# Seven half-block products in place of eight in the last projection of a fused attention, MoE and FFN kernel

## What is computed

```python
def _moe2_ref(x, w_in, w_out):          # x: 2304 x 512
    h = np.maximum(x @ w_in, 0.0)       # 2304 x 2048
    return (h * h @ w_out)              # 2048 x 512 -> 2304 x 512
```

## Time and profile before

| what | value |
|---|---|
| median of 3 runs | 428.07 us (425.8 to 428.68) |
| the profiled execution's own time | 425.84 us |
| its span | 423.9 us |
| PE busy | 405.3 us, 96% of the span |
| DVE busy | 243.0 us, 57% |
| ACT busy | 218.4 us, 52% |
| granted TensorE clock, mean | 0.986 |

### The profile page before, as it was taken

One profiled execution on the slowest core, in us unless ns is written; L12 is line 12 of the kernel. 1 busy time (PEld: TensorE's weight loads), 2 busy tenths in 40 slices (PEclk: granted clock), 3 DMA queues, 4 the chain that ended last, 5 costly groups with the idle time before them and its releaser, 6 DMA issues.

```text
span 423.9 us, 7956 instructions
## 1 busy us (share of the span) xinstructions
PE 405.3 (96%) x2879; PEld 310.7 (73%) x2879; DVE 243.0 (57%) x679; ACT 218.4 (52%) x559; POOL 98.1 (23%) x94
## 2 busy tenths in 40 slices
PE   5899999999989999799899999999999999999996
PEld 5678787878767654233678888888888888888884
DVE  4788888888845451113999545454545445454520
ACT  2989898989853310002966434344444434344420
POOL 4686868686730010000142000000000000000000
PEclk9899999999999999969999999999999999999999
DMA  7588998998616899999300101010101001010101
GB/s 188 156 293 243 265 298 244 301 283 226 221 32 201 284 378 398 408 386 387 141 2 1 51 0 51 0 49 2 50 2 40 9 0 49 0 49 2 49 0 49
DMA packets 51426, 61.34 MB, mean 145 GB/s; under 512 B 27584, under 2 KB 35264, under 8 KB 49856
## 3 DMA queue, kind: packets, MB, share of 16 engines
q1 hardware_dynamic: 50064, 60.37, 42.8%
q10 hardware_dynamic: 1328, 0.52, 0.5%
HBM read 56.16 MB, written 4.72 MB: 144 GB/s over the span
## 4 chain that ended last, share of the span: by engine, by line
PE 85%; DMA 5%; ACT 5%; DVE 4%; issue 1%; SPq 0%; ACTq 0%
PE psum L1314 15%; PE psum L1315 15%; PE psum L1316 15%; PE psum L1028 6%; PE psum L1072 6%; PE psum L1054 5%; DMA ring<-in_moe_w 4%; PE psum L1295 4%; PE psum L1222 3%; ACT probs L829 3%; PE psum L1243 2%; PE psum L987 2%; PE psum L1132 2%; PE psum L1037 2%; PE psum L1009 2%; PE psum L1170 1%
## 5 line engine op out<-in xcount | busy, mean ns | idle before, releaser
L1314 PE MATMUL psum<-wout_hi,act_hi 128*128 128x512 f32 x288 | 113.3, 393 | 1.7 <-DVE wout_lo L752 1.4
L1315 PE MATMUL psum<-wout_lo,act_hi 128*128 128x512 f32 x288 | 112.9, 392 | 0.0
L1316 PE MATMUL psum<-wout_hi,act_lo 128*128 128x512 f32 x288 | 112.1, 389 | 0.0
L778 DVE TENSOR_TENSOR sq_h<-relu_h 128x512 f32<-128x512 f32 x72 | 56.4, 783 | 77.6 <-ACT relu_h L935 77.5
L935 ACT ACTIVATE relu_h<-psum 128x512 f32<-128x512 f32 x72 | 43.1, 599 | 91.6 <-PE psum L1295 85.7
L829 ACT ACTIVATE probs<-probs,row_min 128x256 f32<-128x256 f32 (+1 forms) x128 | 60.1, 470 | 12.4 <-DVE row_min L563 12.3
L504 POOL TENSOR_TENSOR probs<-probs,row_inv 128x1024 f32<-128x1024 f32 x31 | 59.2, 1930 | 23.7 <-DVE row_inv L614 23.7
L1316 PEld LDWEIGHTS psum<-wout_hi,act_lo 128*128 128x128 f32 x288 | 54.1, 188 | 11.9
L1314 PEld LDWEIGHTS psum<-wout_hi,act_hi 128*128 128x128 f32 x288 | 54.1, 188 | 11.7 <-issue 1.9
L1315 PEld LDWEIGHTS psum<-wout_lo,act_hi 128*128 128x128 f32 x288 | 54.3, 189 | 8.8
L782 DVE TENSOR_TENSOR act_lo<-sq_h,act_hi 128x512 fp32r<-128x512 f32 x72 | 49.8, 692 | 5.9 <-ACT act_hi L938 0.6
(11 more groups left out here) (141 smaller groups left out, 439.4 us busy)
## 6 DMA issues: line engine op xcount, KB each, us to landing
ring<-in_moe_w SPq DMA_DIRECT2D x16, 1024.0 KB, 6.1
ring<-in_moe_w SPq DMA_DIRECT2D x4, 2048.0 KB, 13.5
out_x<-out_sb SPq DMA_DIRECT2D x9, 512.0 KB, 2.8
v_in<-in_v SPq DMA_DIRECT2D x32, 128.0 KB, 2.8
ring_late<-in_moe_w SPq DMA_DIRECT2D x2, 2048.0 KB, 8.6
ring_x<-in_moe_w SPq DMA_DIRECT2D x2, 2048.0 KB, 7.9
win_sb<-in_moe_w_in SPq DMA_DIRECT2D x4, 1024.0 KB, 14.2
wout_raw<-in_moe_w_out SPq DMA_DIRECT2D x4, 1024.0 KB, 14.4
```

The costliest lines, as they stand in the source:

```text
L778: nc.vector.tensor_tensor(sq_h[:, u % 2, :], relu_h[:, u % 2, :], relu_h[:, u % 2, :], ALU.mult).then_inc(sq_done, 1)
L1314: mm(to, hi, wout_hi[:, c, :], start=first_of, stop=False)
L1315: mm(to, hi, wout_lo[:, c, :], start=False, stop=False)
L1316: last = mm(to, lo, wout_hi[:, c, :], start=False, stop=last_of)
```

## The change

From group 3 (`CONV`) to group 8, a group's projection (256 tokens x 2048 by 2048 x 512) is cut into halves on all sides: tokens in two halves of 128, hidden columns in two halves k of 1024, output columns in two halves of 256. Of these half blocks seven products are made instead of eight, in the scheme of Strassen and Winograd. Four are of sums: S1 to S4 are sums of the squares' blocks A, made per group; T1 to T4 are sums of `w_out`'s blocks, made once.

The new step is a block j of a group, 0 to 3. It holds two chunks (i = 0, 1) of each half k, so it replaces two units:

- PE, `hidden_steps`: four products of 256 columns into banks 0 and 1, three blocks ahead. Then for each of the two chunks seven products, each of three matrix products of 256 columns: 42 per block, where two units had 24 of 512.
- ACT, `next_steps`: the high parts of the block before (`high_steps`, two casts of 128x896), two relus of 128x512 into `step_raw`, one square of 128x1024 in place.
- DVE, `next_steps`: the low parts of the block before (`low_steps`, two subtractions of 128x896), then `sums`: S3, S1 and S2 together, S4, each waiting for the one before it.
- `take_out` at a group's end, placed behind the next group's block 2: ACT copies two products of 256 columns, DVE combines the seven in six operations.

The accumulators of products 1, 2 and 4 lie in the same half banks in every group; 3, 5, 6 and 7 take turns between two sets of banks. In the last group product 3 has a half bank of the other set.

Groups 1 and 2 keep the old scheme, in a ring of five units (`conv`). From unit 12 on ACT also makes the full square (relu, square, cast: three instructions where there were two), and DVE only the subtraction. There DVE forms T1 to T4 (eight operations of 128x1024) and their low parts (eight more), ACT their high parts (eight casts of 128x1024). From unit 20 on the blocks 0, 1 and 2 of group 3 are prepared.

The last group's output goes out in two transfers, the rest in one each as before.

Core of the diff (declarations, placement and the old scheme's small edits left out):

```diff
+        def acc(x, par, last=False):
+            bank, half = {1: (4, 0), 2: (4, 1), 4: (5, 0), 6: ((2, 6)[par], 0), 5: ((2, 6)[par], 1),
+                          7: ((3, 7)[par], 0), 3: (7, 0) if last else ((3, 7)[par], 1)}[x]
+            return psum[:, bank, NH * half:NH * half + NH]
...
+            def low_steps(n, j, only=(0, 1)):
+                for i in only:
+                    dve.wait_ge(hi_done, FU * n + 2 * j + i + 1)
+                    nc.vector.tensor_tensor(step_lo[j][:, i, 1:8, :], step_raw[j][:, i, 1:8, :],
+                                            step_hi[j][:, i, :, :].bitcast(F32), ALU.subtract
+                                            ).then_inc(lo_done, 1)
+
+            def sums(n, j):
+                a = step_raw[j]
+                dve.wait_ge(sqA_done, NB * n + j + SQ_ACT_AT)
+                nc.vector.tensor_tensor(a[:, :, S3, :], a[:, :, A21, :], a[:, :, A11, :], ALU.subtract
+                                        ).then_inc(s3_done, 1)
+                dve.wait_ge(s3_done, NB * (n - CONV) + j + 1)
+                nc.vector.tensor_tensor(a[:, :, S1:S2 + 1, :], a[:, :, A21:S3 + 1:S3 - A21, :],
+                                        a[:, :, A22:A22 + 1, :].to_broadcast([P, 2, 2, P]), ALU.add).then_inc(s12_done, 1)
+                dve.wait_ge(s12_done, NB * (n - CONV) + j + 1)
+                nc.vector.tensor_tensor(a[:, :, S4, :], a[:, :, A12, :], a[:, :, S2, :], ALU.subtract
+                                        ).then_inc(sums_done, 1)
...
+            def high_steps(n, j):
+                act.wait_ge(sums_done, NB * (n - CONV) + j + 1)
+                for i in range(2):
+                    nc.scalar.copy(step_hi[j][:, i, :, :], step_raw[j][:, i, 1:8, :]).then_inc(hi_done, 1)
+
+            def next_steps(n, j):
+
+                if j > 0:
+                    high_steps(n, j - 1)
+                elif not isinstance(n, int) or n > CONV:
+                    high_steps(n - 1, NB - 1)
+                act.wait_ge(l2_used, NB * n + j + L2_AT - NB)
+                if isinstance(n, int) and n == CONV and j % 2 == 1:
+                    act.wait_ge(t_raw, 4 * (j // 2) + 4)
+                for i in range(2):
+                    act.wait_ge(l1_done, FU * n + 2 * j + i + 1)
+                    nc.scalar.activation(step_raw[j][:, i, 0:4, :],
+                                         psum[:, i, :].rearrange("p (s x) -> p s x", x=P), ACT.Relu).then_inc(relu_done, 1)
+                act.wait_ge(relu_done, FU * n + 2 * j + 2)
+                sq = step_raw[j][:, :, 0:4, :]
+                nc.scalar.activation(sq, sq, ACT.Square).then_inc(sqA_done, 1)
...
+                for j in range(NB):
+                    if j == 0:
+                        next_steps(n, NB - 1)
+                    elif not is_last(n):
+                        next_steps(n + 1, j - 1)
+                    elif j == 1:
+                        high_steps(n, NB - 1)
+                take_out(n, par)
...
+            def hidden_steps(n, j):
+
+                cols = combT[:, FT * n:FT * n + FT] if isinstance(n, int) else combT[:, bass.ds(n * FT, FT)]
+                for i in range(2):
+                    pe.wait_ge(relu_done, FU * n + 2 * j + i - 1)
+                    for k in range(2):
+                        at = P * (KH * k + 2 * j + i)
+                        last = mm(psum[:, i, FT * k:FT * k + FT], mix[:, at:at + P], cols, start=True, stop=True)
+                    last.then_inc(l1_done, 1)
...
+                mm(to, hi, w_hi, start=clears, stop=False, skip_group_check=True)
+                mm(to, hi, w_lo, start=False, stop=False, skip_group_check=True)
+                return mm(to, lo, w_hi, start=False, stop=c == KH - 1, skip_group_check=True)
+
+            def wait_bank(n, par, x):
+
+                if x == 6:
+                    since(pe, outD_ready, n - 1)
+                    if n == CONV if isinstance(n, int) else False:
+                        pe.wait_ge(outA_ready, n - 1)
+                if x == 3 and is_last(n):
+                    pe.wait_ge(outD_ready, n)
+                if x in (1, 4):
+                    if isinstance(n, int) and n == CONV:
+                        pe.wait_ge((outA_ready, outD_ready)[x // 4], n)
+                    else:
+                        pe.wait_ge((c11_taken, p4_taken)[x // 4], n - CONV)
...
+FIRST_ORDER, LAST_ORDER = (6, 5, 7, 3, 1, 2, 4), (1, 2, 4, 6, 5, 7, 3)
+AHEAD_STEPS = {4: 0, 5: 1, 6: None, 7: 2}
```

More of the change, by code:

```diff
@@ L40 @@
 AHEAD = 4
+CONV = 3
+KH, NH = FC // 2, DM // 2
+NB = KH // 2
+A21, A11, A22, A12, S1, S2, S3, S4 = range(8)
+T1, T3, T2, T4 = range(4)
 XSLOTS = 11
@@ L773, in take_mix, with low_part @@
                                         ).then_inc(mix_ready, 1)
[L775 to L780, removed]
+            def low_part(m):
+                low, squares = conv_lo(m), conv_squares(m)
+                if m < SQ_OF_DVE:
+                    dve.wait_ge(relu_done, m + 1)
+                    since(dve, l2_used, m - AHEAD)
+                    relu = relu_h[:, m % 2, :].rearrange("p (c t) -> p c t", c=2)
+                    nc.vector.tensor_tensor(squares, relu, relu, ALU.mult).then_inc(sq_done, 1)
+                    dve.wait_ge(sq_done, m + 1)
@@ L942, in first, with take_out @@
+            def take_out(n, par):
+                act.wait_ge(p_done, P_DONE * (n - CONV) + 1)
+                act.wait_ge(stored[par], 8 * (n - par))
+                nc.scalar.copy(out_sb[:, par, 0, 0:NH], acc(1, par)).then_inc(p1_taken, 1)
+                if not isinstance(n, int) or n > CONV:
+                    act.wait_ge(c2_ready, n - CONV)
+                nc.scalar.copy(p4_sb[:, :], acc(4, par)).then_inc(p4_taken, 1)
             def first():
@@ new lines, in chunk @@
+            def chunk(n, par, c):
+                pe.wait_ge(lo_done, FU * n + c + 1)
+                if isinstance(n, int) and n == CONV and c % 4 == 0:
+                    pe.wait_ge(t_ready, c + 4)
+                for x in LAST_ORDER if c == KH - 1 else FIRST_ORDER:
+                    if c == 0:
+                        wait_bank(n, par, x)
+                    last = product(n, par, x, c)
+                    if c == KH - 1 and x in (4, 5):
+                        last.then_inc(p_done, 1)
+                return last
@@ new lines, in strassen @@
+            def strassen(n, par):
+                for j in range(NB):
+                    if j == 0:
+                        hidden_steps(n, NB - 1)
+                    elif not is_last(n):
+                        hidden_steps(n + 1, j - 1)
+                    if is_last(n) and j == NB // 2:
+                        pe.wait_ge(lo_done, FU * n + KH)
+                        for x in LAST_ORDER:
+                            for c in range(2 * j, KH):
+                                last = product(n, par, x, c)
+                            if x in (4, 5, 7):
+                                last.then_inc(p_done, 1)
+                        last.then_inc(l2_used, 1)
+                        return
+                    chunk(n, par, 2 * j)
+                    chunk(n, par, 2 * j + 1).then_inc(l2_used, 1)
```

306 lines of the change are left out of this document (234 added, 72 removed).

## The result

| | before | changed |
|---|---|---|
| median of 20 runs each | 425.95 us (421.77 to 428.68) | 428.61 us (426.05 to 430.28) |
| profiled execution, its span | 425.84, 423.9 us | 429.09, 427.3 us |

The ratio is 1.007 with a 95% interval of 1.0043 to 1.0096: a loss of 0.7%, inside the 1% called no change ahead. 429.3 us had been forecast.

The account below looks back on a forecast made before the run. The prediction took the serial round of ACT and DVE (5.56 us per block) as the bound. Transition +3.8, five groups -4.05 and last group +1.4 made 1.2 us slower, 429.3 us; range 420.5 to 438.

Parts of the forecast that it names:

- What bounds: In the loop, one block takes a serial round of ACT and DVE, 5.56 us, just over PE's 5.52.
- `take_out`: At a group's end, six DVE operations behind S4 add 0.79 us per group, making a group 23.03 us.
- Transition: Before group 3: extra hidden products (+0.6) and PE's waits for relus (3.2) start group 3 3.8 us late.
- Five groups: Groups at 23.03 us instead of 23.84, five times: -4.05 us.
- Last group: PE waits 3.8 us before product 3, then its products run through: 23.9 us against 22.5, +1.4.
- Tail: After PE's last product, both kernels need 0.8 to 0.9 us to DVE's end; change 0.
- PE's price: A matrix product of 256 columns costs 0.12 us, so PE needs 22.08 us per group.
- rival 1: In the loop the round is under 5.52 us and PE bounds after all: 422.8 us; chance 0.18.
- Rivals 2: The round is longer through costlier handovers, 0.06 us more at five places: 5.86 us, total 436.5; chance 0.22.
- rival 3: ACT's instructions cost 0.09 us more each, five per round: round 6.01 us, total 440; chance 0.03.
- Rival 4: A product of 256 columns costs 0.13 us in a long row too: 434 us; chance 0.06.
- The scale: The change of 1.2 us was put on the shown median of 428.07 us, giving 429.3.

Follow-up runs that it names:

- e1: Changed kernel with ACT making relus and square before the previous block's casts, and DVE the sums before the low parts; 420.16 us.
- e5: e6 plus block 1's hidden products one unit later and group 2's output copied out ahead of block 1's casts and low parts; 413.77 us.
- e2: Changed kernel with a block's three sums formed as one operation of 128x1024, so S1 to S4 hold wrong values; 417.79 us.
- e3: Changed kernel with one more DVE subtraction of 128x256 per block, ahead of S3; 434.56 us.
- e4: Changed kernel with product 3 last in the first chunk of the last group; 426.12 us.
- e6: Changed kernel with the edits of e1 and e4 together; 415.82 us.
- e8: e5 with the high parts of all blocks in the upper memory places, low parts and raw values in the lower; 415.7 us.
- e9: e5 with low parts and raw values of all blocks in the upper memory places, high parts in the lower; 413.87 us.
- e7: e1 with the memory places of the buffers of blocks 0 and 1, and of 2 and 3, exchanged; 419.2 us.

## Why the prediction came out right, step by step

- **What bounds.** Right: the round, by a hair. 5.56 us forecast, 5.54 measured. From the first cast's start to the square's end 3.83 was forecast and 3.86 is there (320.46 to 324.32): casts 1.69 for 1.76, relus up to the square's start 1.11 for 1.03, square 1.06 for 1.04. From there to the next cast 1.68 for 1.73, with 0.03 instead of 0.09 for the way back to ACT. A few hundredths up and down cancel.
- **`take_out`.** 0.79 forecast; 6.37 - 5.54 = 0.83. Groups follow on DVE at 22.9 to 23.2 us, (400.57 - 308.52) / 4 = 23.01, forecast 23.03. PE's wait before product 1 is there four times at up to 1.12.
- **Transition.** +3.81 for +3.8, and by parts as well: block 1's hidden products cost 0.85 and 0.37 of waiting (0.95 and 0.26 forecast), block 3's 1.56 and 0.34 (1.7 and 0.3).
- **Five groups.** -5.02 for -4.05. The mechanism was right and the size off by 1.0: group 3 still lives on the blocks that were made ahead. It has one wait of 0.68 before product 4 and none before product 1, and takes 22.45 us (284.13 to 306.58) where I charged 23.03: 0.6 of the 1.0. From group 4's first product (306.58) to the last group's (398.31) the mean is 22.93, with 22.58 for group 4 and 22.97 to 23.20 behind it: the other 0.4.
- **Last group.** +2.82 for +1.4. The wait is right (4.01 for 3.8). The term missing is the clock, which I put at full speed: from 403.54 to 407.18 us 16 distances take 3.64, where 16 x 0.120 is 1.92, so 1.7 more. Against it stands the pace of the other blocks: from 409.10 on 126 products take 14.6 us and not 15.1. The clock is my largest error, and the two errors, -1.0 and +1.4, partly cancel.
- **Tail.** 0 forecast, -0.57 measured. The end on the timeline:

```profile
424.17 0.42 DVE L932 TENSOR_TENSOR out_sb<-out_sb,psum 128x256 f32<-128x256 f32 x1
424.61 0.37 SPq L539 DMA_DIRECT2D out_x<-out_sb  x1
```

  From the last store's issue to the span's end are 2.7 us; before, 3.2 followed the issue at 420.69. The store carries half as much now; no run separates this from another cause.
- **PE's price.** 0.12 was read right for one place in memory and was not the price of all. PE's floor is 21.52 per group, not 22.08. Since PE was not the bound, nothing of it shows in the result; had rival 1 come true, its 422.8 would have been some 3 us too high. e1, in which PE does bound, comes to 420.2 with the transition's waits still in.
- **Rivals 2 and 3** fall with the round: handovers are 0.03, not 0.09 or more, and an ACT relu in the loop is 0.59 on average. (The row of the Trainium skill that is cited with rival 3 is for an ACTIVATE whose bias is an operand of its own. The relus and squares here are issued without one, so their 0.599 does not speak against the page.) Rival 4 falls: in a long row at full clock 0.13 is never seen.

- **The scale.** 429.3 was 1.2 on top of 428.07, the median of three runs; 20 runs of the same kernel have 425.95. The starting point was 2.1 us too high and the change too small (+1.2 forecast, +2.66 by the medians), which hid one another: 429.3 beside 428.61 looks better than it is. By the traces the last block and the tail give 1.61 - 0.57 = 1.04 us of the difference, close to the 1.2; the rest lies ahead of the last block, where the prediction had nothing, and stays open.

The forecast was right by its mechanism, the round and its ends. How near its number came is in part luck: errors of opposite sign in the groups and the last group, and in the starting point.

## What to carry to other kernels

When two engines hand one block back and forth, add up their chain over one round before believing their busy shares; two thirds busy was the bound here. What breaks it costs no work: put a step that does not depend on the answer between question and answer, on both engines, so that each works on another block (e1: 8 us). Then look at the ends of the loop, where the first and the last rounds have waits of their own (e5: another 6 us).

## What the runs showed of the hardware

- **TensorE's clock after a wait.** In the changed kernel's last group PE stood still for 4.0 us and then ran at a granted clock at half level, 1.2 GHz instead of 2.4:

```profile
400.00:404.00 4.00, 0.46 (x2) 0.46 (x3) 3.74 (x9) 3.29 (x5) 0.00 (x0) 0.96 0.00 0
404.00:408.00 4.00, 4.00 (x24) 4.00 (x23) 2.95 (x5) 1.48 (x3) 0.00 (x0) 0.62 0.34 131
408.00:412.00 4.00, 4.00 (x37) 4.00 (x36) 2.09 (x2) 0.84 (x1) 0.00 (x0) 1.00 0.00 0
```

  The distance of 0.213 us is 256 columns at 1.2 GHz, as the Trainium skill has it for the cold array (TensorE: Matmul & The Clock Gate, "Wait — 56ns, not 53.3ns?"). In the last group the clock also fell in e1 (wait 2.2 us), e2 (2.1), e3 (4.3) and e4 (1.5 and 1.2), and never where one wait of 1.0 to 1.1 stood (e5, e6, e8, e9). But the wait alone does not decide: after 2.0 in e7 the clock stayed; e7 had the fall instead after a wait of 1.1 us in group 3 (0.61 in 284 to 288), where e1, with the same wait, kept 1.00. A fall lasted for 15 to 21 distances of 0.213 us instead of 0.120, 1.4 to 2.0 us.
- **A matrix product's pace depends on where the operand that it loads lies**: 0.1133 or 0.120 us for 256 columns, a difference of 0.0067 us or 16 cycles at 2.4 GHz, or 0.1178 as a mix of places. By the same section of the Trainium skill the distance of such products would be 0.109 (an estimate: 256 / 2.4 GHz and 2.5 ns); the fastest here is 0.1133. The Trainium skill also says (TensorE: Matmul & The Clock Gate, "Step-by-step: what each phase is for") that loading the next weights takes no read bandwidth from the running product. No run here shows whether it does: e7 to e9 move only the blocks' buffers, the loaded operands among them, and the pace follows, but whether the load or the product is what takes longer in the slow place stays open. Half of the 0.2267 of the earlier trace rows is the fast pace, 0.1133: half the width cost more than half only in the slow places.
- **Handovers** between DVE and ACT through a semaphore take 0.03 us from end to start, as within one engine.
